# A three-stage attention and mixture-of-experts kernel: when W_in is loaded and split, and which banks the last attention outputs use

## The reference

```python
def _attn_ref(q, k, v, phi):
    a = softmax(phi, axis=2)                       # over the positions
    k_m = np.einsum('bhsm,bhsd->bhmd', a, k)
    v_m = np.einsum('bhsm,bhsd->bhmd', a, v)
    attn = softmax(np.matmul(q, k_m.transpose(0, 1, 3, 2)) / 8.0)
    return np.matmul(attn, v_m)

def _moe_ref(x, w_in, w_out):
    h = x @ w_in
    g = h * (1.0 / (1.0 + np.exp(-1.702 * h)))
    return g @ w_out

def _moe2_ref(x, w_gate, w_output_gate, w1, w2):
    e_idx = np.argmax(x @ w_gate, axis=1)          # one expert per token
    for e in range(8):
        h = np.maximum(x[e_idx == e] @ w1[e], 0.0)
        out[e_idx == e] = gate * eom * (h @ w2[e])
```

## Time and profile before

| | |
|---|---|
| median of 3 runs | 1436.13 us (1427.64 to 1436.95) |
| the profiled execution | 1435.18 us, span 1433.5 us |
| granted TensorE clock, mean | 0.984 |
| PE busy | 1363.0 us, 95% of the span |
| VectorE, ScalarE, POOL busy | 662.7, 423.1, 519.8 us |
| the chain that ended last | PE 87%, DMA 6%, VectorE 2% |
| read from and written to HBM | 146.03 and 100.45 MB |

### The profile page before, as it was taken

How to read it: one execution, slowest core, us unless ns; L and a number is a source line. 1 busy time by engine, 2 the same in 40 slices (tenths; PEclk the granted TensorE clock), 3 DMA queues, 4 the chain that set the end, 5 groups by cost and what they waited for, 6 DMA issues and landing times.

```text
span 1433.5 us, 26261 instructions
## 1 busy us (share of the span) xinstructions
PE 1363.0 (95%) x7922; PEld 1100.0 (77%) x7923; DVE 662.7 (46%) x1363; ACT 423.1 (30%) x762; POOL 519.8 (36%) x617
## 2 busy tenths in 40 slices
PE   5777799999999999999999999999899999999996
PEld 4555478888888888888888888887778888888885
DVE  4777732334343353433434344335554455445442
ACT  2444332222222232222322223223233333333322
POOL 1121384435344444344343443201423334333331
PEclk8999899999999999999999999999999999999999
DMA  8999745755756546565465653336773597649871
GB/s 223 299 306 304 238 131 205 204 184 191 197 184 191 205 161 183 168 184 199 147 182 173 178 205 133 55 127 209 240 227 97 149 270 220 202 111 263 253 229 55
DMA packets 164287, 275.35 MB, mean 192 GB/s; under 512 B 20068, under 2 KB 56693, under 8 KB 164229
## 3 DMA queue, kind: packets, MB, share of 16 engines
q1 hardware_dynamic: 103540, 196.89, 43.4%
q10 hardware_dynamic: 47408, 45.63, 13.4%
q0 software_dynamic: 13280, 32.09, 7.3%
HBM read 146.03 MB, written 100.45 MB: 172 GB/s over the span
## 4 chain that ended last, share of the span: by engine, by line
PE 87%; DMA 6%; DVE 2%; SPq 2%; issue 1%; ACT 1%; ACTq 0%; POOL 0%; DVEq 0%; POOLq 0%
PE ps L633 27%; PE ps L667 27%; PE ps L737 15%; PE ps L708 14%; DMA ph<-in_phi 4%; DMA qraw<-in_q 1%; SPq L410 1%; PE ps L677 1%; PE ps L593 1%; DMA cq<-ch 1%; PE ps L581 0%; PE ps L611 0%; PE ps L567 0%; PE ps L552 0%; DVE xs L1124 0%
## 5 line engine op out<-in xcount | busy, mean ns | idle before, releaser
L633 PE MATMUL ps<-xs,W 128*128 (+1 forms) x1728 | 419.2, 392 | 1.9 <-DVE xs L1124 1.9
L667 PE MATMUL ps<-W,gs 128*128 128x512 f32 x1728 | 415.0, 389 | 0.1
L633 PEld LDWEIGHTS ps<-xs,W 128*128 128x128 f32 x1728 | 324.2, 188 | 73.8 <-issue 4.1
L667 PEld LDWEIGHTS ps<-W,gs 128*128 128x128 f32 x1728 | 324.3, 188 | 67.7 <-DVE gs L1179 0.5
L1177 DVE TENSOR_TENSOR gate<-ps,gate 128x512 f32<-128x512 f32 x144 | 99.6, 692 | 371.0 <-ACT gate L893 370.5
L737 PE MATMUL ps<-W,chT 128*128 (+1 forms) x936 | 222.1, 394 | 7.1 <-issue 4.1
L893 ACT ACTIVATE gate<-ps 128x512 f32<-128x512 f32 x144 | 86.3, 599 | 471.6 <-PE ps L633 459.4
L708 PE MATMUL ps<-W,cx 128*128 (+1 forms) x936 | 218.7, 389 | 0.7 <-DVE cx L1274 0.7
L737 PEld LDWEIGHTS ps<-W,chT 128*128 128x128 f32 x936 | 177.6, 190 | 46.3 <-issue 9.1
L708 PEld LDWEIGHTS ps<-W,cx 128*128 128x128 f32 x936 | 175.5, 188 | 37.7 <-issue 1.3
L1492 POOL CAST whi<-raw 128x512 fp32r<-128x512 f32 x128 | 85.1, 665 | 316.9 <-DMA raw<-in_moe_w 316.9
(11 more groups left out here) (157 smaller groups left out, 921.8 us busy)
## 6 DMA issues: line engine op xcount, KB each, us to landing
W<-expert_scratch SPq DMA_DIRECT2D x24, 2048.0 KB, 10.9
raw<-in_moe_w SPq DMA_DIRECT2D x128, 256.0 KB, 2.8
expert_scratch<-whi SPq DMA_DIRECT2D x128, 256.0 KB, 2.5
expert_scratch<-raw SPq DMA_DIRECT2D x128, 256.0 KB, 2.8
cq<-ch ACTq DMA_DIRECT2D x156, 128.0 KB
crec<-record_scratch POOLq DMA_DIRECT2D x164, 64.0 KB
kvm<-in_k SPq DMA_DIRECT2D x32, 288.0 KB, 7.4
kvm<-in_v SPq DMA_DIRECT2D x32, 288.0 KB, 9.0
```

Of the source, the lines that this page charges most:

```text
L633: mm = pe.matmul(ps[:, f % 2, :], W[:, col:col + P], xs[:, bass.ds(x0 + (x_lo * K1 + c) * T, T)], start=(c == 0 and w_lo + x_lo == 0), sto ...
L667: mm = pe.matmul(ps[:, 2 + s, :], gs[:, f % 2, g_lo, s * P:(s + 1) * P], W[:, col:col + DM], start=(f == 0 and g_lo + w_lo == 0), stop=(f ...
```

## The change

In the attention stage only the first four chunks of W_in are loaded and split: those for hidden columns 0 to 511 (k = 0), of all four quarters of the inputs. The other 12 come after the hand-over. In the first tile SP loads, and POOL splits, alternately a part of W_out and one of W_in (k = 1, 2, 3), and at the end the last four of W_out. The load of x for tile 1, ahead of the loads of W_out before, now stands behind the first eight of the parts. POOL starts on these 28 chunks only when all of x_lo for tile 0 is done. The waits of PE follow: `mm1(0, f)` waits for its chunks every fourth step, `mm2(0, f)` for its part. The output halves of the last two groups get banks of their own (4/5, 2/3, 6/7, 4/5), so that no half waits for the copy of the half just before it.

```diff
@@ SP @@
-            def load_w(n, i, src):
+            def load_w(n, src):
                 wait(sp, s_wlo, n - 1)
-                sp.dma_start(raw[:, i, :], src).then_inc(s_wraw[i], 16)
+                sp.dma_start(raw[:, n % 2, :], src).then_inc(s_wraw[n % 2], 16)
+            def w_in_part(c, k):
+                return w_in_v[:, c * F1 + k * CH:c * F1 + (k + 1) * CH]
...
-                if not isinstance(g, int) or g + 1 < NG:
-                    load_w(g + 1, 1 - u, w_in_v[:, bass.ds((g + 1) * CH, CH)])
+                if isinstance(g, int) and g + 1 < K1:
+                    load_w(g + 1, w_in_part(g + 1, 0))
...
             load_x(0)
-            for f in range(2):
-                load_w(C1 + f, f, w_out_v[f])
+            load_w(K1, w_out_v[0])
+            load_w(K1 + 1, w_in_part(0, 1))
...
                 if first:
-                    load_x(t + 1)
-                    for f in range(2, C1):
-                        load_w(C1 + f, f % 2, w_out_v[f])
+                    for k in range(1, 4):
+                        for c in range(K1):
+                            f = 4 * (k - 1) + c
+                            if f:
+                                load_w(K1 + 2 * f, w_out_v[f])
+                                load_w(K1 + 2 * f + 1, w_in_part(c, k))
+                        if k == 1:
+                            load_x(t + 1)
+                    for f in range(12, C1):
+                        load_w(16 + f, w_out_v[f])
                     sp.wait_ge(s_wlo, 2 * C1)
@@ PE @@
-            def out_half(g, r, i):
+            def out_half(g, r, i, bank=4):
...
-                wait(pe, s_xo, 2 * g + i)
+                if isinstance(g, int) and g >= NG - 2:
+                    pe.wait_ge(s_xo, 2 * (NG - 2) + (1 if g == NG - 1 else 0))
+                else:
+                    wait(pe, s_xo, 2 * g + i)
...
-                    pe.wait_ge(s_wlo, C1)
+                if isinstance(t, int) and t == 0 and f % 4 == 0:
+                    pe.wait_ge(s_wlo, K1 + 2 * f)
...
-                out_half(NG - 2, (NG - 2) % 4, i)
+                out_half(NG - 2, (NG - 2) % 4, i, (4, 2)[i])
             mm1(0, 1)
             for i in range(2):
-                out_half(NG - 1, (NG - 1) % 4, i)
+                out_half(NG - 1, (NG - 1) % 4, i, (6, 4)[i])
...
-                    pe.wait_ge(s_wlo, C1 + f + 1)
+                    pe.wait_ge(s_wlo, K1 + 2 * f + 1 if f < 12 else 17 + f)
@@ POOL @@
-            for n in range(C1):
-                split_w_in(n, n % 2)
+            for c in range(K1):
+                split_w_in(c, c, 0)
...
                 if first:
-                    for i in range(16):
-                        split_w(C1 + i, i % 2, SLOT + i * CH)
+                    pool.wait_ge(b_xlo, K1)
+                    for k in range(1, 4):
+                        for c in range(K1):
+                            f = 4 * (k - 1) + c
+                            split_w(K1 + 2 * f, 0, SLOT + f * CH)
+                            split_w_in(K1 + 2 * f + 1, c, k)
+                    for f in range(12, C1):
+                        split_w(16 + f, f % 2, SLOT + f * CH)
```

More of the change, by code:

```diff
@@ L425, in _ @@
             load_qkv(1, 0, 1)
-            load_w(0, 0, w_in_v[:, 0:CH])
+            load_w(0, w_in_part(0, 0))
             sp.wait_ge(b_setup, 2)
@@ L450, in _ @@
                     sp_group(4 * m + (3 + j), 2 * m + (3 + j) // 2, (3 + j) % 4)
-            for g in range(NG - 5, NG - 1):
+            for g in range(NG - 5, NG - 2):
                 sp_group(g, g // 2, g % 4)
@@ L547, in out_half @@
                     wait(pe, s_vbd, g + 1)
-                wait(pe, s_xo, 2 * g + i)
+                if isinstance(g, int) and g >= NG - 2:
+                    pe.wait_ge(s_xo, 2 * (NG - 2) + (1 if g == NG - 1 else 0))
+                else:
+                    wait(pe, s_xo, 2 * g + i)
                 for pair in range(2):
                     rows = slice(pair * 64, pair * 64 + 64)
-                    mm = pe.matmul(ps[:, 4 + pair, 0:HS], vbd[rows, r, :], pT[rows, i * HS:(i + 1) * HS],
+                    mm = pe.matmul(ps[:, bank + pair, 0:HS], vbd[rows, r, :], pT[rows, i * HS:(i + 1) * HS],
                                    start=True, stop=True, tile_position=(pair * 64, 0))
@@ L838, in q_out, with x_out @@
                     act.copy(q_flat[:, 512:QA * D], ps[:, 2:4, :].rearrange("p k n -> p (k n)")[:, 512 - P:]).then_inc(s_qT, 1)
-            def x_out(g, b, u, i):
+            def x_out(g, b, u, i, bank=4):
                 wait(act, s_o, 2 * g + i + 1)
@@ L844, in x_out @@
                     wait(act, s_xst[u], 16 * b)
-                act.copy(xo[:, u, :, i * HS:(i + 1) * HS], ps[:, 4:6, 0:HS]).then_inc(s_xo, 1)
+                act.copy(xo[:, u, :, i * HS:(i + 1) * HS], ps[:, bank:bank + 2, 0:HS]).then_inc(s_xo, 1)
                 if i == 1:
@@ L885, in _ @@
             exp_scores(NG - 1)
-            x_out(NG - 2, B - 1, 0, 1)
+            x_out(NG - 2, B - 1, 0, 1, 2)
             def g_step(t, f):
@@ L995, in _ @@
             g_step(0, 0)
-            x_out(NG - 1, B - 1, 1, 0)
+            x_out(NG - 1, B - 1, 1, 0, 6)
             x_out(NG - 1, B - 1, 1, 1)
@@ L1469, in split_w, with split_w_in @@
                 pool.tensor_tensor(lo, raw[:, i, :], hi.bitcast(F32), ALU.subtract).then_inc(s_wlo, 1)
-            def split_w_in(n, i):
-                c, f = n // 4, n % 4 * 4
+            def split_w_in(n, c, k):
+                i = n % 2
                 by_f = raw[:, i, :].rearrange("p (f n) -> p f n", f=4)
-                hi, lo = w_in_sb[:, f:f + 4, 0, c, :], w_in_sb[:, f:f + 4, 1, c, :]
+                hi, lo = w_in_sb[:, 4 * k:4 * k + 4, 0, c, :], w_in_sb[:, 4 * k:4 * k + 4, 1, c, :]
                 hold(pool, s_wraw[i], 8 * (n - i) + 16)
```

## The result

The changed kernel took 1451.6 us (median of 5 runs, 1447.25 to 1457.93). The kernel before, run beside it, took 1436.13 us (median of 5, 1423.59 to 1439.55). The ratio is **1.0123, with a 95% interval of 1.008 to 1.0166**: a loss of 1.2%, small but clear of none, as forecast in sign and near the forecast in size (1455 us said, range 1442 to 1466). By the medians the change costs 15.5 us, by the ratio 17.7 (11 to 24), where 18.9 were forecast (1455 against 1436.13).

The account below looks back on a forecast made before the run. Transfers bound the attention stage, TensorE the rest, with POOL's serial stream at most 3 us ahead of need. On 1435.2 us: -11.3 (T0) + 30.4 (stream) - 1.4 (slack) + 1.9 (clock) = +19.6, said 1455 us, range 1442 to 1466.

Parts of the forecast that it names:

- T0: Start of the MLP's first matmul on PE: 11.3 us earlier (8.0 from loads, 3.3 from quiet POOL), at 160.7.
- first rival: POOL's stream after T0 or the expert chunks run faster, scatter in time, all is gain: 1422.6 us; chance 0.08.
- The hand-over: Last phi to T0: with POOL quiet, VectorE's six stretched two-input operations get back 3.3 us.
- The ten loads: W_in loads ahead of group 15's in the attention stage: leaving them out saves 8.0 us, at most 8.6.
- The banks: Last groups' output halves: first W_out matmul 1.3 us earlier relative to T0, then lost in PE's wait for the scatter.
- The stream: POOL's 28 splits after T0 end at T0 + 70.8, near 231.5, where before the last ended at T0 + 40.4.
- To the scatter and through it: POOL's padding and 29 expert chunks unchanged, 134.7 us for the chunks; tile 0's record scatter starts at 369.9, lands 377.4.
- slack: Before, tile 0's scatter was ready for PE's step 0 of W_out in tile 2 with 1.4 us to spare.
- The wait: PE stands 30 us before step 0 of W_out in tile 2 (the place), until tile 0's scatter lands.
- The clock behind the wait: After PE's idle stretch the first 12 matmuls run at half clock, 1.9 us more, once.
- A shorter wait: POOL's stream is quicker by some 10 to 28 us in all: 1425 to 1445 us; chance 0.07.
- The attention stage does not shrink: VectorE binds there, T0 falls by 3.3 us only, the loss is 8 larger: 1463 us; chance 0.08.

Follow-up runs that it names:

- scatter5: Changed kernel with a tile's record scatter issued ahead of the 6th expert chunk of the next tile, not the 14th; 1417.32 us, ratio 0.9876 to the kernel before.
- scatter9: Changed kernel with a tile's record scatter issued ahead of the 10th expert chunk of the next tile, not the 14th; 1432.0 us, ratio 1.0004 to the kernel before.
- before_scatter5: Kernel before with only the record scatter moved ahead of the 6th expert chunk, from the 14th; 1432.55 us, ratio 0.9982 to the kernel before.
- banks_only: Kernel before with only the output banks of the last two groups changed; 1438.63 us, ratio 1.0021 to the kernel before.
- split_only: Changed kernel with the output banks of before put back; 1449.29 us, ratio 1.0104 to the kernel before.
- no_xlo_wait: Changed kernel without POOL's wait for x_lo, so it splits already loaded parts during the hand-over; 1449.89 us, ratio 1.013 to the kernel before.
- extra_w_out: Changed kernel with ten extra, unread loads of contiguous W_out chunks in the attention stage, nothing split; 1461.85 us, ratio 1.0218 to the kernel before.
- extra_w_in: Changed kernel with ten extra, unread loads of W_in chunks (2 KB pieces) in the attention stage, nothing split; 1461.54 us, ratio 1.0217 to the kernel before.

## Why the prediction was right, and where its terms were off

**The mechanism** was right in every step that sets the time: T0 earlier, the stream's end later by more, the scatter behind it, the copies of `rec` released by a DMA, one wait of PE, half clock after it, nothing of it given back. `scatter5` and `scatter9` show that the wait is the loss. With the wait gone, the change gains 17.0 us by the medians, 18 by the ratio (11 to 25); the forecast's first rival had 12.6. That rival was some 4 us short: T0 gained 14.0 us by the means where 11.3 was forecast, and it had no term for the clock at T0. Both are taken up below.

**T0.** Forecast 160.7, 11.3 us earlier. The profile has 152.4, 19.6 earlier, which looks like a large miss. Most of it is none, since T0 varies between executions of the same code. All profiled executions that have the hand-over of the kernel before or that of the changed kernel:

| T0 of one execution each | us |
|---|---|
| W_in loaded in the attention stage (before, `before_scatter5`, `banks_only`) | 171.98, 175.58, 164.91; mean 170.8 |
| a quarter of W_in (after, `scatter5`, `split_only`, `scatter9`) | 152.41, 162.94, 154.17, 157.66; mean 156.8 |

Within a row the spread is some 10.5 us, though the code up to T0 differs in nothing that acts there. The difference of the means is 14.0, with a standard error of some 4 from the spread. The profiled execution of after was 4.4 us earlier than its mean, and 4.4 us below the median of its runs. So of the 19.6 us in the pair of traces, some 5.6 belong to the spread. The forecast's own range for T0, 160 to 163, made no room for it, and of the four only `scatter5` fell inside: so it is in part luck that the total came out in its range. What varies is the time up to the last phi: 154.08, 157.39 and 146.61 with W_in; 138.15, 148.65, 138.66 and 143.40 without, and 144.10 in `no_xlo_wait`.

*The hand-over*, in contrast, repeats well: from the last phi to T0 17.90, 18.19 and 18.30 us with POOL's splits beside it, 14.26, 14.29 and 14.26 in the changed kernel, `scatter5` and `scatter9`, and 15.51 in `split_only`. This last is not for want of the banks: VectorE waited 1.30 us for PE there, and 0.79 in `extra_w_out`, which has the banks and took 15.01. The means of the first three and the next four differ by 3.6 us, and `no_xlo_wait` gives 3.2; the forecast's 3.3 from six operations was right. *The ten loads* are then 14.0 - 3.6 = 10.4 us by the mean T0s and about 10 by the kernels with extra loads, where 8.0 was forecast with 8.6 as its upper bound. A third way gives less. The eleven groups from the fifth phi to the last took 108.8, 111.3 and 101.3 us with W_in (mean 107.2), 94.1, 93.4, 98.3, 98.8 and 100.4 without (97.0, `no_xlo_wait` included), and 105.2 and 101.8 with the extra loads (103.5): 10.2 us between the first two means, and only 6.5 for the ten extra loads. VectorE's busy time in these stretches is 81 to 83 us in all ten kernels, so it is not that POOL's splits stretched VectorE there; what differs are its phi waits, 10.0 to 21.8 us with W_in and 4.2 to 11.0 without. If a term was too small it is this one, but with a standard error of 4 us none of these ways can tell 10 or 6.5 from 8. The bound counted only the bytes at the rate of the window, 0.86 us a chunk. Without these loads the window has 319 GB/s instead of 306, so what stays may also move a little faster, which that bound left out.

**The banks.** Forecast: 1.3 us earlier, then lost in the wait. `banks_only` has 1.5 us earlier in a single pair and no change of the time; `split_only` has the same 26.2 us wait as the whole change. The size of the gain is not settled, since the way from T0 to the first W_out matmul varies by more: 15.4 and 17.0 us in two executions of the same code.

**The stream.** Forecast T0 + 70.8; it was T0 + 70.2, 70.3 and 70.2 in the changed kernel, `scatter5` and `scatter9`, + 71.7 in `split_only`, and + 68.8 and 70.9 in the kernels with extra loads. The sum came out better than its parts, which is luck. The forecast had 66.1 for the chunks and 4.7 for two delays. The timeline of POOL has 26 periods of 2.46 us and a last split of 1.9, together 65.9, and one delay of 1.8 us, at the load of x:

```profile
173.97 0.61 POOL L1484 CAST W<-raw 128x512 fp32r<-128x512 f32 x1 [2.29 <-DMA raw<-in_moe_w_out]
```

That chunk starts 4.27 us after the last and not 2.46, so the period with the delay in it closes the sum: 65.9 + 4.3 = 70.2. The delay before the first chunk was put in by mistake: the first two parts are loaded when POOL is let go, and it begins at T0 itself (152.42). What makes up for most of it is the longer period, 2.46 for 2.39, some 2 us over all of them.

**Parts late in tile 0?** Forecast none, with 3 to 5 us of margin. PE's waits from 150 to 366 us are 1.9 us for `pT`, 1.1 us for x_lo ahead of T0 and 0.5 us for kmT: none for a part.

**To the scatter and through it.** Forecast 134.7 + 3.7 us for padding and expert chunks, unchanged (138.4 from the end of the splits); 136.2 came. This stretch of the same code took 134.4 us in `split_only`, 137.5 in `no_xlo_wait`, 138.0 and 137.2 in the two with extra loads and 141.5 in `banks_only`, so the 2.2 us are within its own variation and no effect of the change. The landing was put at 3.5 us, with 3.9 as the most that the trace of before allowed. Now it can be read: 362.71 to 367.20, 4.49 us; 4.35 in `banks_only` (351.18 to 355.53); 4.05 in `scatter9`, and 4.4 to 4.5 in four others. So the 4.5 of the earlier trace rows was the better witness for the changed kernel. For the execution of before the bound of 3.9 still holds, and with it the slack was at least 361.07 - 354.74 - 3.9 - 1.4 = 1.0 us, near the forecast's 1.4. What made the term 0.4 and not 1.0 is that the scatter took at least 0.6 us longer to land after the change.

**The wait.** Forecast 30 us; it was 26.2. PE reached the place at 342.3, T0 + 189.9, 2.1 later than the forecast's T0 + 187.8 (348.5 - 160.7), and went on at 368.6, T0 + 216.2, 1.9 sooner than the forecast's T0 + 218.1. Only the second of these moves the time. The first is the clock, next.

**The clock behind the wait.** Forecast +1.9 us; 4.36 against 2.88 in the profile is 1.5. In six other kernels with such a wait the first 12 matmuls took 4.67 to 5.46 us, and PE was 1.8 to 2.9 us late by then or one group later, most of all in `banks_only`, after only 4.3 us of idle. The windows of after at the place (columns as in the earlier trace rows):

```profile
368.00:370.00 2.00, 1.36 (x3) 1.16 (x4) 1.18 (x2) 1.24 (x3) 0.56 (x1) 0.50 0.26 29
```

The granted clock is 0.50, the 1.2 GHz level, after 26 us of idle, and 1.00 again from 372 us on.

**The clock at T0.** This the forecast did not have. The first 12 matmuls of the MLP took 4.68 us before and 4.60 in the profiled execution of the changed kernel, at granted clocks down to 0.50, but 3.01 or 3.02 in `scatter5`, `scatter9`, `split_only` and `extra_w_in`, at 1.00. Before, and in `no_xlo_wait`, the clock is at 0.50 when T0 comes: there VectorE is stretched by POOL's splits and PE is busy for 0.13 us or not at all in the last 2 us, for 0.7 to 0.8 us in the quiet kernels. From T0 to the first W_out matmul it was 15.4, 17.0 and 13.9 us with those splits, 13.1, 13.2, 13.1 and 12.7 in the quiet kernels that kept the clock, and 16.2 and 16.0 in the two quiet ones (the changed kernel and `split_only`) where it fell to 0.50 somewhere between the two matmuls. Why it fell in these two and not in the others is open. In the changed kernel the wait hides this; without the wait it counts. PE passed the place at T0 + 189.1 and 190.7 in the kernel before and `before_scatter5`, and at T0 + 186.8 in `scatter5`, 3.1 us sooner than their mean. What the banks bring is in these 3.1 us, too. With the 14.0 us of T0 that makes 17.1 us, beside the 17.0 that `scatter5` gained by the medians; with an error of 4 us on the first, so near a match is luck.

**The sum with what was measured**: -14.0 (T0) + 29.8 (stream) - 2.2 (to the scatter) - 0.4 (slack and landing) + 1.5 (clock) = +14.7, beside +15.5 by the medians and +17.7 by the ratio. The T0 in it has a standard error of 4 us and the other terms are those of one pair, so that it comes this near is in part luck. The forecast's +19.6 lies 4.9 us above: 2.7 by T0, 2.2 by the expert chunks, 0.6 by the stream, 0.4 by the clock, and the slack goes the other way by 1.0. None of the first four is larger than the spread of its own term.

**The rivals.** *No new wait, faster* fell, since the stream ran as forecast; `scatter5` is what it would have given, at 1417 us. *A shorter wait* (10 to 28 us quicker) fell: the wait was 26.2 us, forecast 30. *The attention stage does not shrink* fell: the period went from 9.89 to 8.55 us in the pair, and from 9.7 to 8.8 by the means of the eleven groups. VectorE's own work in it is 7.4 us, so this rival is what would stop a further step of the kind.

**What stays open**: what makes the attention stage take 138 us in one execution and 149 in the next, to the last phi; whether the layout of the loads has a part of a few us; why the clock fell behind T0 in two of the quiet kernels; and 3 us of the profile pair in the expert stage.

## What to carry to other kernels

Where work is moved off a stage bound by transfers, the question is whose queue it lands in and what stands behind it there. POOL was a third busy (36%) and yet at its limit, because its stream is serial, a tile's 16 expert chunks take 16 x 4.64 = 74 us, and an instruction near their end held back the emptying of TensorE's PSUM banks. Follow that queue to the first thing another engine needs, and compare the two arrival times; here the slack was 1.0 us or a little more, and 30 us of added stream became 26 us of wait. Then move the needed instruction ahead in the queue in the same edit: it turned a loss of 15 us into a gain of 17.

A second lesson is on reading pairs of traces. A stage that varies by 10 us between executions can't be sized from two of them; take the traces of all kernels with the same code there, and prefer differences between two events in one trace (phi to T0 within 1.3 us here, T0 to the stream's end within 2.9). Even these are not all steady: from the end of the splits to the scatter it was 134.4 to 141.5 us.

## What the runs showed of the hardware

- The attention stage, bound by transfers (DMA share 1.05), ends within a range of some 10 us from one execution to the next, for the same code: last phi at 154.1, 157.4 and 146.6; 138.2 and 148.7. The cause is open.
- Ten loads of 0.262 MB in 2 KB pieces 32 KB apart, or contiguous: 1461.5 and 1461.9 us for the kernel, each with some 10 us to either side, so no difference that can be told. One such load costs 0.65 us by the eleven groups of the traces, 1.0 by the medians and 1.35 by the ratios, in a stage with the DMA engines full. The Trainium skill (DMA: Bandwidth & Descriptors, Latency and other measured facts) tells of copies that are slower at row pitches of 2 MiB and more than at 512 KiB; no run here had such a pitch.
- Two-input VectorE operations beside POOL's splits: three pieces of x_lo took 4.24 us for 1.88 alone, and POOL's subtractions beside them 1.66 and 1.59 for 1.28; the whole hand-over 3.2 to 3.6 us more.
- An indirect scatter landed 4.05 to 4.54 us after its issue began, in seven kernels, and in the kernel before in at most 3.9.
- TensorE's granted clock went to 0.50 during an idle stretch of 4.3 us as during one of 26 us. PE was late by 2.9 us after the short one (`banks_only`) and by 1.5 after the long one, so a longer idle stretch did not cost more clock.
